# Attention stage: instruction orders of all five engines rewritten around one head pair, with two value products instead of three

## The chip, the cores and the metric

One core of a Trainium2 chip runs the whole program; the metric is the device time of one execution in microseconds. TensorE appears as PE (its weight loads as PEld), VectorE as DVE, ScalarE as ACT, GpSimd as POOL and SyncE, which only issues DMAs here, as SP. A difference counts where it is larger than 0.2%.

## The reference

The program is attention with a score threshold, a mixture of experts and a token-mixing layer, one after the other. The change is in the attention alone (4 batches x 8 heads, 576 tokens, 64 features a head):

```python
scores = scale * np.matmul(q, k.transpose(0, 1, 3, 2))
thresh = np.max(scores, axis=-1, keepdims=True) - tau
scores = np.where(scores >= thresh, scores, -1000000000.0)
scores = scores - np.max(scores, axis=-1, keepdims=True)
attn = np.exp(scores)
attn = attn / (np.sum(attn, axis=-1, keepdims=True) + 1e-09)
return np.matmul(attn, v).astype(np.float32)
```

## The kernel before

The 32 heads are worked as 16 pairs of two heads. A pair has nine tiles of 128 query rows by 576 keys: u = 0 to 7 are four full blocks of each head in turn, and u = 8 holds the last 64 rows of both heads. Each tile passes through these steps.

- **scores** (L459, PE): q and k are split into a high and a low part that are stacked along the 128 rows of the array, so that a tile is four products of 288 columns (eight in the tile of both heads). The result lies in one of three PSUM places `s_bank`. A tile may be written only when the mask of the tile three before it is done (`s_mask`).
- **row_max** (L376, DVE), **exp** (L514, ACT, into `e_ring`, two buffers), **mask** (L391, DVE, into `p_ring`, nine tiles, with the row's sum).
- **sum_eps** and **recip** (L404, L409, DVE) turn three tiles' sums into factors at once.
- **norm** (L320, POOL) multiplies a tile of `p_ring` by its factor.
- **"t"** (L472, PE) transposes the first 512 keys of a tile; **"k"** (L476, PE) transposes the last 64 keys, four tiles (or one) in a group, with 64 other keys that are thrown away; ACT copies the result (L546) into `p_t`.
- **"pv"** (L483, PE) multiplies by v: query columns 0 to 255, 256 to 511, and the last 64 in a third product. **"r"** (L488, PE) turns the result to token rows and multiplies by the gates; ACT copies it to `x_tmp`, and SP writes it out.

The groups "t", "k", "pv", "r" share two PSUM banks in turn, so each waits until the group two before it has been copied (`s_free`).

The stacked operands come by a path of their own, one pair ahead of their use. POOL scales and splits q and k of pair p+2 in five parts that stand between the norms of pair p (`split`: L292 scale, L303 and L306 high and low part of q, L311 and L314 of k). SP waits for the low parts and then copies them inside SBUF into `q_st` (`stack_q`, four copies, L193) and `k_st` (`stack_k`, four copies, L200). The first tile of scores of pair p+2 waits for all eight.

The order on each engine is fixed in the code. A step k of the loop body issues scores k+7, exp k+6, mask and row maximum near k+6, norm k+5 and the groups of tile k; the same rule serves every tile. During the last pairs POOL also splits eight pieces of the first expert's weights (`split_piece`, L53 and L55).

## Time and profile before

| | us |
|---|---|
| median of 3 runs | 906.8 (906.3 to 906.98) |
| profiled execution: time, span | 913.87, 912.1 |
| attention, from the start to the last copy of logits | 327.1 |
| PE busy in the span | 820.3 (90%) |
| 100 to 250 us: PE, DVE, ACT, POOL busy | 148.60, 117.50, 114.95, 94.67 of 150 |

The median stands 7.1 us, or 0.8%, below the profiled execution; differences are taken inside the trace and put on the median. In a timeline row the columns are the start, the time from there to the end of the last instruction merged into the row, engine and line, the operation with its operands, the count, and in brackets the idle time ahead of it and what ended it. PE matmuls overlap, so from one group's start to the next group's start is what a group costs; the row's own time is longer. In a row of stretches the columns are the stretch, its length, the busy time of PE, PEld, DVE, ACT and POOL with their counts, the granted clock, the share of the 16 DMA engines and GB/s. Names in the rows follow memory: `xs_nat` and `u` are also the places of the value result.

### The profile page before, as it was taken

The numbers are of one execution on the slowest core, as the hardware profiler recorded it, in microseconds if no ns is written. First come the engines' busy times: TensorE is split into PE (matmuls) and PEld (weight loads), VectorE is DVE, ScalarE is ACT, GpSimd is POOL, SyncE is SP. The second block draws the span as 40 slices with busy tenths as digits, with TensorE's granted clock in tenths as the row PEclk, the third lists the DMA queues.
The fourth block names the chain that finished last, engine by engine and source line by source line (L and its number), as shares of the span: only waits on it lengthen the run. The fifth ranks groups of instructions, "written<-read, shape, count | busy, mean of one in ns | idle before, by whom it ended". The sixth has DMA issues, their size and how long they took to land. (4 is left out here: it accounts for less than half of the span.)

```text
span 912.1 us, 17390 instructions
## 1 busy us (share of the span) xinstructions
PE 820.3 (90%) x5424; PEld 696.5 (76%) x5425; DVE 448.8 (49%) x1044; ACT 395.4 (43%) x669; POOL 519.8 (57%) x462
## 2 busy tenths in 40 slices
PE   1989999999999832989999999999578999999998
PEld 1778887888888621767888888888457899999998
DVE  3867877778777445112121221122156865656622
ACT  2667777778777540111222121222066634434400
POOL 3556665666588901963799779999238522503200
PEclk9899999999999975998999999999779999999999
DMA  9977567756766151675655545572121110110101
GB/s 225 327 172 176 145 157 177 177 144 167 175 151 159 56 198 56 221 226 188 230 184 173 184 138 175 181 266 73 51 89 41 36 64 19 41 53 1 37 16 52
DMA packets 81441, 123.17 MB, mean 135 GB/s; under 512 B 28352, under 2 KB 41920, under 8 KB 81408
## 3 DMA queue, kind: packets, MB, share of 16 engines
q1 hardware_dynamic: 71280, 99.34, 37.7%
q10 hardware_dynamic: 6656, 12.13, 4.2%
q0 software_dynamic: 3472, 11.28, 4.1%
q8 instruction: 19, 0.31, 0.1%
q14 instruction: 14, 0.11, 0.0%
HBM read 70.55 MB, written 23.86 MB: 103 GB/s over the span
## 5 line engine op out<-in xcount | busy, mean ns | idle before, releaser
L320 POOL TENSOR_SCALAR p_ring<-p_ring,rsum 128x576 f32<-128x576 f32 x144 | 107.1, 750 | 93.4 <-DVE rsum L409 93.2
L459 PE MATMUL psum<-k_st,q_st 128*128 128x288 f32 x640 | 125.0, 323 | 26.5 <-DMA q_st<-q_split 17.3
L376 DVE TENSOR_REDUCE negmax<-psum 128x1 f32<-128x576 f32 x144 | 108.4, 753 | 73.6 <-PE psum L459 72.4
L459 PEld LDWEIGHTS psum<-k_st,q_st 128*128 128x128 f32 x640 | 94.3, 198 | 39.3 <-issue 26.8
L997 PE MATMUL psum<-w_split,h_hi 128*128 x352 | 118.3, 408 | 4.1 <-DVE h_lo L1061 3.2
L976 PE MATMUL psum<-w_split,x_hi 128*128 x352 | 118.2, 407 | 4.1 <-issue 2.2
L391 DVE SCALAR_TENSOR_TENSOR p_ring<-psum,thresh,e_ring 128x576 f32<-128x576 f32 x144 | 116.8, 811 | 5.0 <-PE psum L476 2.3
L903 POOL TENSOR_TENSOR w_split<-w_raw,w_split 128x1024 fp32r<-128x1024 f32 x48 | 115.4, 2403 | 4.0
L514 ACT ACTIVATE e_ring<-psum,negmax 128x576 f32<-128x576 f32 x144 | 107.7, 748 | 19.3 <-DVE negmax L376 16.4
L546 ACT COPY p_t<-psum 128x512 f32<-128x512 f32 (+1 forms) x192 | 107.7, 561 | 16.1 <-PE psum L472 12.2
L472 PE MATMUL psum<-ident,p_ring 128*128 128x128 f32 x576 | 89.0, 278 | 4.5 <-POOL p_ring L320 4.0
L483 PE MATMUL psum<-p_t,v_sb 128*64 128x256 f32 (+1 forms) x960 | 89.3, 332 | 0.5 <-ACT p_t L546 0.5
L1183 POOL TENSOR_TENSOR stage<-g,xs_nat 128x512 f32<-128x512 f32 (+1 forms) x20 | 27.3, 1366 | 108.5 <-ACT xs_nat L1389 108.5
L1316 PE MATMUL psum<-tok_hi,z_hi 128*128 128x288 f32 x288 | 86.2, 299 | 1.5 <-DVE z_lo L1226 1.5
L1316 PE MATMUL psum<-tok_lo,z_hi 128*128 128x288 f32 x288 | 84.9, 295 | 0.0
L1316 PE MATMUL psum<-tok_hi,z_lo 128*128 128x288 f32 x288 | 84.8, 294 | 0.0
L1030 ACT CAST h_hi<-psum 128x1024 fp32r<-128x1024 f32 x22 | 22.4, 1017 | 142.1 <-PE psum L985 125.0
L997 PEld LDWEIGHTS psum<-w_split,h_hi 128*128 128x128 f32 x352 | 68.5, 195 | 18.9 <-issue 4.8
L976 PEld LDWEIGHTS psum<-w_split,x_hi 128*128 128x128 f32 x352 | 67.7, 193 | 18.9 <-issue 4.9
L483 PEld LDWEIGHTS psum<-p_t,v_sb 128*64 128x64 f32 x960 | 54.2, 137 | 28.0 <-ACT p_t L546 7.8
L472 PEld LDWEIGHTS psum<-ident,p_ring 128*128 128x128 f32 x576 | 67.9, 141 | 9.2 <-issue 4.8
L997 PE MATMUL psum<-w_split,h_lo 128*128 x176 | 70.8, 402 | 0.0
(182 smaller groups left out, 1563.1 us busy)
## 6 DMA issues: line engine op xcount, KB each, us to landing
w_raw<-w_dram SPq DMA_DIRECT2D x48, 512.0 KB, 3.6
k_st<-k_split SPq DMA_DIRECT2D x64, 288.0 KB, 5.0
q_st<-q_split SPq DMA_DIRECT2D x60, 144.0 KB, 2.5
xs_dram<-stage SPq DMA_DIRECT2D x23, 256.0 KB
xs_nat<-xs_dram ACTq DMA_DIRECT2D x22, 256.0 KB
ys_dram<-y_nat ACTq DMA_DIRECT2D x22, 256.0 KB, 2.1
k_nat<-k_t_dram SPq DMA_DIRECT2D x16, 288.0 KB, 4.3
q_nat<-q_t_dram SPq DMA_DIRECT2D x16, 288.0 KB, 4.6
```

Source lines behind the costliest of these rows:

```text
L320: pl.tensor_scalar(t, t, rsum[:, k % BODY:k % BODY + 1], 1.0, ALU.mult, ALU.mult).then_inc(s_norm, 1)
L376: dve.tensor_reduce(negmax[:, k % 3, 0:1], s_bank[k % 3][:, :, 0:HALF], AX.XY, ALU.max, negate=True).then_inc(s_max, 1)
L391: dve.scalar_tensor_tensor(out=p_ring[:, k % RING, :].rearrange("p (a b) -> p a b", a=2), in0=s_bank[k % 3][:, :, 0:HALF], scalar=thresh[: ...
L459: mm = pe.matmul(bank[:, x, 0:HALF], lhs, key[:, HALF * x:HALF * x + HALF], start=(j == 0), stop=(j == len(terms) - 1))
L472: mm = pe.transpose(bank[:, t * P:t * P + P], p_ring[:, k % RING, t * P:t * P + P], ident[:])
L483: mm = pe.matmul(bank[D * h:D * h + D, 0:n], v_sb[m % 2][:, h, t, :], p_t[arg % 2][:, h, t, 0:n], start=(t == 0), stop=(t == KT - 1))
L514: act.activation(e_ring[:, k % 2, :].rearrange("p (a b) -> p a b", a=2), s_bank[k % 3][:, :, 0:HALF], ACT.Exp, bias=negmax[:, k % 3, 0:1], ...
L546: act.copy(dst, src).then_inc(s_free, 1)
L903: lo = pl.tensor_tensor(w_lo[:, (m + 1) % 2, r // 4, part], raw[:, r % 4, :], w_hi[:, (m + 1) % 2, r // 4, part].bitcast(F32), ALU.subtract)
L976: mm = pe.matmul(ph[:, half, :], a[:, c, :], rhs.rearrange("p o n -> p (o n)"), start=(n == 0), stop=(n == len(terms) - 1))
L997: mm = pe.matmul(py, a[:, f, :], rhs.rearrange("p o n -> p (o n)"), start=(n == 0), stop=(n == len(terms) - 1))
L1316: mm = pe.matmul(mix_bank(b, q), a[:, k, c * P:c * P + P], w[:, k, half], start=(t == 0 and i == 0), stop=(t == ST - 1 and i == len(terms) ...
```

## The change

The order of every engine is written out for one pair (`pair(i, m)`), instead of a step that serves every tile.

- The tile of both heads' last rows is now u = 0 and comes first. Its queries join columns 0 to 255, so "pv" is one product of 320 columns and one of 256, and one copy less.
- The keys of head 0's tiles start 64 places later in memory, and tiles of both heads lie next to each other in `p_ring`. One transposition of 128 columns takes the last 64 keys of head 0 and of head 1. A pair has six "k" transpositions in two groups instead of nine in three. The last row block of v is padded with zeros for the other head.
- For this k comes with its last 64 keys repeated ahead: `k_nat`, `k_split` and `k_st` have 640 columns instead of 576. The k split on POOL, the load of k and the four stack copies grow by one ninth.
- `e_ring` has three buffers. Small tiles, `turn` and `x_t` move to memory that other stages use later.
- The weight pieces stand at other places in POOL's last four pairs.

```diff
-    e_ring = sb("e_ring", [P, 2, S], F32)
+    e_ring = sb("e_ring", [P, 3, S], F32)
-    k_st = [sb(f"k_st{m}", [P, 2, 2, S], F32R) for m in range(2)]
+    k_st = [sb(f"k_st{m}", [P, 2, 2, REM + S], F32R) for m in range(2)]
-    k_split = sb("k_split", [P, 2, S], F32R)
+    k_split = sb("k_split", [P, 2, REM + S], F32R)
+    ORDER = (("t", 0), ("pv", 1), ("t", 1), ("t", 2), ("t", 3), ("r", 1), ("k", 0), ("t", 4), ("t", 5), ("pv", 0),
+             ("k", 1), ("t", 6), ("r", 0), ("t", 7), ("t", 8))
+    BEHIND = (("pv", 1), ("r", 1))
...
+        def values(i, m, a):
+            bank = bank_of(i, m, "pv", a)
+            if a == 0:
+                pe.wait_ge(s_v[m % 2], 64 * i + 64)
+            for t in range(KT):
+                for h in range(2):
+                    moving = p_t[a][:, h, t, :] if t < FULL else p_k[a]
+                    mm = pe.matmul(bank[D * h:D * h + D, 0:COLS[a]], v_sb[m % 2][:, h, t, :], moving,
+                                   start=(t == 0), stop=(t == KT - 1))
+            mm.then_inc(s_filled, 1)
...
+            if parts:
+                split(i + 1, m, 1)
+            piece(0)
+            if here:
+                norm(i, m, 5)
+            if parts:
+                split(i + 1, m, 2)
+            if here:
+                norm(i, m, 6)
+                norm(i, m, 7)
+            if parts:
+                split(i + 1, m, 3)
+            piece(1)
+            if here:
+                norm(i, m, 8)
+            if parts:
+                split(i + 1, m, 4)
...
+            if u < 2 and not (isinstance(i, int) and 2 * i + m == 0):
+
+                dve.wait_ge(s_filled, (number(i, 0, "k", 0) if m else number(i - 1, 1, "k", 0)) + 1)
...
+        pair(ITER - 2, 0, pieces=((2, 0),))
+        pair(ITER - 2, 1, pieces=((2, 1),))
+        pair(ITER - 1, 0, pieces=((0, 2), (1, 3), (2, 4)))
+        pair(ITER - 1, 1, ahead=False, pieces=((0, 5), (1, 6), (2, 7)))
```

POOL, in the loop, from the high part of q of pair p+2 to the low part of its k; the rows on `p_ring` are norms, and the first norm after L306 is the one that needs the last factors of pair p. Before:

```order
L303 TENSOR_SCALAR q_split<-u 128x576 [waits s_qst1]
L277 REGISTER_ALU
L320 TENSOR_SCALAR p_ring<-p_ring,rsum 128x576 [waits s_rsum]
L306 TENSOR_TENSOR q_split<-u,q_split 128x576 [waits s_qhi]
L320 TENSOR_SCALAR p_ring<-p_ring,rsum 128x576 [waits s_rsum]
L311 TENSOR_SCALAR k_split<-k_nat 128x576 [waits s_kraw0,s_kst1]
L320 TENSOR_SCALAR p_ring<-p_ring,rsum 128x576 [waits s_rsum]
L314 TENSOR_TENSOR k_split<-k_nat,k_split 128x576 [waits s_khi]
```

The same place now:

```order
L307 TENSOR_SCALAR q_split<-u 128x576 [waits s_qst0]
L324 TENSOR_SCALAR p_ring<-p_ring,xs_nat 128x576 [waits s_rsum]
L310 TENSOR_TENSOR q_split<-u,q_split 128x576 [waits s_qhi]
L281 REGISTER_ALU
L324 TENSOR_SCALAR p_ring<-p_ring,xs_nat 128x576 [waits s_rsum] x2
L315 TENSOR_SCALAR k_split<-k_nat 128x640 [waits s_kraw1,s_kst0]
L324 TENSOR_SCALAR p_ring<-p_ring,xs_nat 128x576 [waits s_rsum]
L318 TENSOR_TENSOR k_split<-k_nat,k_split 128x640 [waits s_khi]
```

In the first list the norm ahead of L306 is tile 6 and waits for the pair's last factors; in the second it is tile 5, so the low part of q no longer stands behind them. Three norms and both parts of k still do.

DVE at the turn from one pair to the next, where the last three factors of a pair are made (`sums`, `rsum`, `negmax` and `thresh` are all named `xs_nat` after the change). Before, from the row maximum of the next pair's first tile:

```order
L376 TENSOR_REDUCE negmax<-psum 128x1 [waits s_scores]
L391 SCALAR_TENSOR_TENSOR p_ring,sums<-psum,thresh,e_ring 128x576 [waits s_thr,s_exp]
L381 TENSOR_REDUCE thresh<-negmax 128x1 [waits s_max]
L375 REGISTER_ALU
L376 TENSOR_REDUCE negmax<-psum 128x1 [waits s_scores]
L404 TENSOR_REDUCE rsum<-sums 128x3 [waits s_mask]
L390 REGISTER_ALU [waits s_thr,s_exp]
L391 SCALAR_TENSOR_TENSOR p_ring,sums<-psum,thresh,e_ring 128x576 [waits s_filled]
L408 REGISTER_ALU
L409 RECIPROCAL rsum<-rsum 128x3 [waits s_sum]
```

Now:

```order
L405 TENSOR_REDUCE xs_nat<-psum 128x1 [waits s_scores]
L420 SCALAR_TENSOR_TENSOR p_ring,xs_nat<-psum,xs_nat,e_ring 128x576 [waits s_thr,s_exp]
L410 TENSOR_REDUCE xs_nat<-xs_nat 128x1 [waits s_max]
L419 ISA [waits s_thr,s_exp]
L420 SCALAR_TENSOR_TENSOR p_ring,xs_nat<-psum,xs_nat,e_ring 128x576 [waits s_filled]
L430 TENSOR_REDUCE xs_nat<-xs_nat 128x3 [waits s_mask]
L404 REGISTER_ALU
L405 TENSOR_REDUCE xs_nat<-psum 128x1 [waits s_scores]
L434 REGISTER_ALU
L435 RECIPROCAL xs_nat<-xs_nat 128x3 [waits s_sum]
```

The next pair's first mask, which waits for a "k" group on PE (`s_filled`), has moved ahead of the second row maximum, and the reciprocal now stands behind both.

PE from the first tile of scores of the next pair to the "k" group for which that mask waits, as it is now:

```order
L516 MATMUL psum<-k_st,q_st 128x288 [waits s_mask,s_kst0,s_qst0]
L516 MATMUL psum<-k_st,q_st 128x288 x7
L534 MATMUL psum<-ident,p_ring 128x128 [waits s_norm,s_free]
L534 MATMUL psum<-ident,p_ring 128x128 x3
L563 MATMUL psum<-u,stage 128x137 [waits s_free]
L563 MATMUL psum<-u,stage 128x137 x2
L516 MATMUL psum<-k_st,q_st 128x288 [waits s_mask]
L516 MATMUL psum<-k_st,q_st 128x288 x3
L545 MATMUL psum<-ident,p_ring 128x128 [waits s_norm,s_free]
L545 MATMUL psum<-ident,p_ring 128x128 x3
```

The eight products of the first tile carry the waits for `k_st` and `q_st`; before the change that tile had four, and its first mask did not stand behind a "k" group that comes later than its own scores.

## Rows read from the trace of the kernel before

**Rows 1.** Busy time by stretch, the steady middle of the attention.

```profile
100.00:250.00 150.00, 148.60 (x1300) 122.87 (x1299) 117.50 (x351) 114.95 (x216) 94.67 (x124) 1.00 0.68 166
```

**Rows 2.** Timeline of PE, parts of one pair; 197.92 and 215.96 open pairs.

```profile
197.92 0.77 PE L459 MATMUL psum<-k_st,q_st 128*128 128x288 f32 x4
...
199.40 0.77 PE L459 MATMUL psum<-k_st,q_st 128*128 128x288 f32 x4
200.01 0.60 PE L472 MATMUL psum<-ident,p_ring 128*128 128x128 f32 x4
200.44 0.60 PE L476 MATMUL psum<-ident,p_ring 128*128 128x128 f32 x4
...
209.49 2.38 PE L483 MATMUL psum<-p_t,v_sb 128*64 128x256 f32 x20
...
212.62 0.80 PE L483 MATMUL psum<-p_t,v_sb 128*64 128x64 f32 x20
...
213.77 1.30 PE L459 MATMUL psum<-k_st,q_st 128*128 128x288 f32 x8
214.91 0.86 PE L488 MATMUL psum<-turn,xs_nat 128*128 x6
215.60 0.60 PE L472 MATMUL psum<-ident,p_ring 128*128 128x128 f32 x4
215.96 0.77 PE L459 MATMUL psum<-k_st,q_st 128*128 128x288 f32 x4
```

**Rows 3.** Timeline of SP: the last of four copies to k_st.

```profile
209.88 1.50 SPq L200 DMA_DIRECT2D k_st<-k_split  x1
```

**Rows 4.** Instructions on k_st, 195 to 216 us: landing of its four copies.

```profile
DMA to landing us min/median/max: 3.1/4.7/5.5
```

**Rows 5.** Timeline of POOL in the same pair.

```profile
202.23 0.75 POOL L320 TENSOR_SCALAR p_ring<-p_ring,rsum 128x576 f32<-128x576 f32 x1 [2.17 <-DVE rsum L409]
...
205.06 0.68 POOL L311 TENSOR_SCALAR k_split<-k_nat 128x576 fp32r<-128x576 f32 x1
205.71 0.75 POOL L320 TENSOR_SCALAR p_ring<-p_ring,rsum 128x576 f32<-128x576 f32 x1
206.43 1.42 POOL L314 TENSOR_TENSOR k_split<-k_nat,k_split 128x576 fp32r<-128x576 f32 x1
```

**Rows 6.** Timeline of DVE in the same pair.

```profile
201.06 0.15 DVE L404 TENSOR_REDUCE rsum<-sums 128x3 f32<-128x6 f32 x1
201.12 0.81 DVE L391 SCALAR_TENSOR_TENSOR p_ring<-psum,thresh,e_ring 128x576 f32<-128x576 f32 x1
...
201.86 0.17 DVE L409 RECIPROCAL rsum<-rsum 128x3 f32<-128x3 f32 x1
...
215.11 0.76 DVE L376 TENSOR_REDUCE negmax<-psum 128x1 f32<-128x576 f32 x1 [0.72 <-PE psum L459]
215.78 0.81 DVE L391 SCALAR_TENSOR_TENSOR p_ring<-psum,thresh,e_ring 128x576 f32<-128x576 f32 x1
```

**Rows 7.** Timeline of PE: first scores of pairs 2, 3 and 15.

```profile
52.66 0.79 PE L459 MATMUL psum<-k_st,q_st 128*128 128x288 f32 x4 [3.15 <-DMA k_st<-k_split]
...
71.64 0.80 PE L459 MATMUL psum<-k_st,q_st 128*128 128x288 f32 x4 [0.77 <-DMA k_st<-k_split]
...
288.91 0.78 PE L459 MATMUL psum<-k_st,q_st 128*128 128x288 f32 x4
```

**Rows 8.** Timeline of POOL: one weight piece, and the attention's last instruction.

```profile
300.59 1.04 POOL L53 TENSOR_SCALAR w_split<-stage 128x1024 fp32r<-128x1024 f32 x1
...
304.06 0.74 POOL L320 TENSOR_SCALAR p_ring<-p_ring,rsum 128x576 f32<-128x576 f32 x1
...
326.88 0.23 POOL L325 COPY lg<-x_tmp 128x45 f32<-128x45 f32 x1 [9.01 <-ACT x_tmp L546]
```

**Rows 9.** Timeline of PE: a long wait near the end.

```profile
300.04 0.63 PE L472 MATMUL psum<-ident,p_ring 128*128 128x128 f32 x4 [1.55 <-POOL p_ring L320]
```

**Rows 10.** Busy time by stretch, just after that wait.

```profile
300.50:304.00 3.50, 3.50 (x18) 2.95 (x18) 2.35 (x7) 2.50 (x4) 3.42 (x3) 0.51 0.02 5
```

More of the change, by code:

```diff
@@ L332, in pool @@
             split(0, 1, part)
-        for k in range(AHEAD_M):
-            norm(0, k)
-        def step(i, k, more=True, last=False, piece=None):
-            m, u = k // TILES, k % TILES
-            if u < PARTS and (m < 2 or more) and not last:
-                split(i + (m + 2) // 2, m % 2, u)
-            if piece is not None:
-                split_piece(pl, w, feed, 0, piece)
-            if not (last and k + AHEAD_M >= BODY):
-                norm(i, k + AHEAD_M)
-            for m in range(2):
-                if k == TILES * m + TILES + 4:
-                    take_logits(i, m, ALL_GROUPS - PER_ITER * i if last and m == 1 else ROWS_DONE[m])
@@ L406, in recip @@
[L406 to L422 removed]
+                out=p_tile[u].rearrange("p (a b) -> p a b", a=2), in0=s_bank[u % 3][:, :, 0:HALF],
@@ L491, in tensor, with bank_of @@
-        pe.wait_ge(s_zero, 4)
-        for k in range(AHEAD_S):
-            scores(0, k)
-        def step(i, k, groups, last=False):
-            if not (last and k + AHEAD_S >= BODY):
-                scores(i, k + AHEAD_S)
-            for n, what, arg, m in groups[k]:
-                group(i, n, what, arg, m, k)
+        def bank_of(i, m, what, arg):
+            n = number(i, m, what, arg)
+            if not (isinstance(n, int) and n < 2):
+                last = isinstance(n, int) and n >= ALL_GROUPS - len(BEHIND)
+                pe.wait_ge(s_free, n if last else n - 1)
+            return misc[number(0, 2 + m % 2, what, arg) % 2] if not isinstance(n, int) else misc[n % 2]
@@ L501, in tensor @@
+        pe.wait_ge(s_zero, 5)
+        pair(-1, 1, past=False, here=False)
         pe.wait_ge(s_ident, 16)
         pe.wait_ge(s_turn, 16)
[L503 to L546 removed]
@@ L1571 @@
     q_t = inputs["q"].transpose(0, 1, 3, 2).reshape(pairs, 2, 64, SEQ)
+    k_t = inputs["k"].transpose(0, 1, 3, 2).reshape(pairs, 2, 64, SEQ)
     gates = np.concatenate([inputs["moe_w_gate"], inputs["moe_w_local"]], axis=1).reshape(DC, P, EXPERTS + 1)
```

529 lines of the change are left out of this document (324 added, 205 removed).

## The prediction

> **What bounds the kernel now.** I read the busy times by stretch first. In the steady middle PE is busy 148.60 of 150 us, the next engine 117.50 [rows 1], so PE's order sets the pace there. The attention is over at 327.1 us (326.88 + 0.23) [rows 8]; nothing behind it is touched, so the whole effect lies ahead of that point. Busy PE rows overlap, so I then read the timeline of one pair from start to start. Pairs open at 197.92 and 215.96: a pair takes 18.04 us [rows 2].
>
> What PE needs for a pair when nothing waits follows from the steps there: a tile of scores 0.61 (199.40 to 200.01), the tile of both heads 1.14 (213.77 to 214.91), a "t" group 0.36 ahead of scores and 0.43 ahead of another group, a three-block "r" 0.69 [rows 2]. A value product of 256 columns takes 2.38 and one of 64 columns 0.80 in time busy, their steps about 0.07 less [rows 2]. Before, that is 8 x 0.61 + 1.14 + 9 x 0.38 + "k" 0.85 + "r" 1.15 + values 2 x 2.31 + 0.73 = 16.8. So 1.2 us of the 18.04 are hand-overs between engines.
>
> The second thing to see is the path on which a pair's operands come, though hardly a wait stands on it now. The low part of k is done at 207.85 (206.43 + 1.42) [rows 5]. The last of the four copies to k_st is issued at 209.88 [rows 3] and lands 5.5 us later [rows 4], at 215.38. The pair opens at 215.96. The slack is about 0.5 us in 18. From the split's end to the landing it is 7.53 us.
>
> **The change on PE.** Values become 320 and 256 columns. From 0.80 and 2.38 a column costs 0.0082 us, so 320 columns take 2.31 + 0.52 = 2.83, and the two 5.14 instead of 5.35: 0.2 saved. "k" groups have six transpositions instead of nine: 0.25 saved. PE's need falls to 16.35 us. The new order puts scores between groups wherever a bank must be copied. I walked it through with the steps above, with copies of 0.6 on ACT and 0.74 for a mask: no wait on PE over 0.3 us at any place but one. By PE alone a pair would take about 16.6 us. The third exponential buffer, the smaller key copies and one copy less on ACT, which is busy 114.95 of 150 [rows 1], are behind PE: nothing. Their cover is ACT's idle quarter; without it the copies would be on the path at 0.3 us a pair.
>
> **The place where it stays: a loop through the operands.** I count from the first tile of scores of pair p+1. All steps are in the new order, with durations of before.
> - The scores' tile of both heads now comes first. Its row maximum starts 1.34 later (213.77 to 215.11) [rows 2, 6].
> - PE goes on: "t" at 1.14, "r" of three blocks at 1.57, scores at 2.27, the four-transposition "k" group at 2.88, done 0.60 later [rows 2]. The first mask waits for this group, whose reading it would overwrite: 3.54 with the hand-over. By its own inputs it could start at 3.1.
> - Mask 0.74 (201.12 to 201.86), small sum 0.06, row maximum 0.67 (215.11 to 215.78) [rows 6]: the reciprocal that frees the last three factors of pair p starts at 5.03. POOL's norm follows 0.37 after its start (201.86 to 202.23) [rows 5, 6]: 5.40.
> - POOL now has two norms at 0.72 (205.71 to 206.43), the high part of k at 0.65, longer by a ninth, 0.73, a norm 0.72, the low part 1.42, longer by a ninth, 1.58 [rows 5]: 9.87. The waiting norms hold up the split behind them, and with it SP's copies.
> - The copies take 7.53 for 576 columns. Landings run from 3.1 after the first issue (made at 207.87, as soon as the split ends) to 215.38: 4.4 us for three copies, 1.47 each [rows 3, 4]. A ninth on four is 0.65. The q copies, which now come earlier because the low part of q stands ahead of the waiting norm, no longer share the queue in the first microsecond: back up to 0.65. I take a net +0.3: 7.8 (bounds 7.5 and 8.2).
> - With 0.1 for the last hand-over the next pair opens 17.8 us after this one (17.5 to 18.2).
>
> The same sum for before: first norm of the last three at 4.31 (197.92 to 202.23) [rows 2, 5], split done at 9.93, copies 7.53, hand-over 0.1: 17.56, just under the 18.04 that PE takes. So the change takes PE's part from 18.04 to 16.6, finds the loop at 17.8, and PE will stand about 1.2 us at each pair's first scores. Gain: 0.24 us a pair.
>
> For the longer copies the nearest page speaks for less. By the Trainium skill, DMA: Bandwidth & Descriptors, section Where 436 GB/s comes from, copies inside SBUF are bounded by a fabric of 435 GB/s; the ninth (131 KB) would then take 0.3 us rather than 0.65. Rows 4 decide, with 288 KB in 1.47 us, which is 200 GB/s counted once.
>
> **Ends.** Start: pair 2 opens at 52.66 after 3.15 us of waiting for k_st [rows 7], since everything loaded by then shares the queue. Three stacks of k longer by 0.65 and four loads of k longer by a ninth come ahead of it, 0.65 to 2.3 us. I take +1.5; nothing that PE saves in the first two pairs survives this wait. Pair 3 opens at 71.64, after another wait for k_st [rows 7]; it follows pair 2 by the same loop in both kernels, 19 us. Middle: from 71.64 to 288.91 are 12 pairs in 217.3 us [rows 7]; 12 x 17.8 = 213.6: -3.7. End: from 288.91 to 327.1 are 38.2 us. A weight piece costs POOL 3.47 (300.59 to 304.06) [rows 8]. Now from the last pair's opening PE needs 11.7 to the eighth tile's scores; POOL's piece 4 ends at 16.65, and behind it stand five norms, two more pieces and another norm until the last: 16.65 + 6 x 0.72 + 2 x 3.47 = 27.9. On that norm hang the second "k" group and four more groups (2.9, with their copies), the value product with its copy (3.0), "r" with its copy and the logits (1.7 to 2.2): 36.0, and 0.4 for a clock that may have fallen. 38.2 - 36.4 = -1.8.
>
> Sum: +1.5 - 3.7 - 1.8 = -4.0, inside the trace 912.1 to 908.1; on the median 906.8 - 4.0 = 902.8, and I say 903.
>
> **Rivals.**
> - *A, the forecast, 0.52.* Loop of 17.5 to 18.05 us; 899 to 907.
> - *B, the loop is not closed, 0.20.* If the copies land in under 7 us, or the norms come earlier than I walked, PE sets the pace. At 16.6: 12 x 1.2 = 14.4 more, 888.5. For it: the walk has steps of 0.1 to 0.4 that could shrink. Against it: every large term is a measured row. Half way (17.2) is 895.5.
> - *C, slower, 0.17.* The same loop, 18.3 us or more, where it exceeds what PE took before. It decides from 18.2: 12 x 0.5 more than A is 909. The copies at their bound of 8.2 and the mask 0.1 later suffice. For it: at pair 3 the wait came even with the shorter copies [rows 7]. Against it: the queue is free of q copies.
> - *D, the clock, 0.11.* After one wait of 1.55 us [rows 9] the granted clock stood at 0.51, the level of 1.2 GHz, for 3.5 us [rows 10]; with every group at twice its length that costs up to 1.7 us. The wait of 3.15 us at pair 2 was followed by none. If PE stands 1.2 us in each pair, the clock may fall again and again; only what exceeds PE's slack of 1.2 us a pair, and what lies in the loop's first 3.5 us, counts: about 0.9 each. From four falls it undoes the gain; in all twelve pairs it gives 903 + 11 = 914. The Trainium skill, TensorE: Matmul & The Clock Gate, section A second HAM failure mode, says that frequent short idle times between groups can make the clock swing between both levels: that speaks for D. The trace agrees in one place of three.
> - That the two value products alone bring nothing is part of A: 0.45 us less PE work a pair is invisible while the loop sets the pace.
>
> **How the numbers follow.** The likeliest is A at 903, own range 899 to 907. Faster than before by over 0.2%, which is 1.8 us and about what a measurement can tell, means under 905.0: 0.40 of A's 0.52, all of B, 0.02 of C and D: 0.62. Within 0.2%: 0.10 of A, 0.08 of C and D: 0.18. Slower: 0.20. From 889 to 910 about 0.15 is left out, half of it B at full strength, half D and the far end of C.
>
> **What the new profile would show.** Right: a pair opens every 17.8 us; ahead of its first scores PE stands about 1.2 us, put down to the DMA of k_st; the busy share of PE falls to about 92%; the value row has 320 columns at about 2.9 us. The first norm of a pair's last three starts 5.4 us after the next pair's opening, the low part of k ends at 9.9, the last copy lands at 17.7. Wrong, by B: no DMA wait there and 16.6 a pair. By C: the same wait with 18.2 or more. By D: the granted clock at 0.5 in the middle slices. What would upset the sum most is a term of the loop that I have 0.3 us wrong, since it counts 12 times.

## The result: 0.4% slower, and the profile after

Before 905.84 us (11 runs, 903.3 to 909.1), after 908.76 us (11 runs, 906.2 to 912.4); the ratio is 1.0038 [1.0021, 1.0056]. I had said 903.

Two executions of later experiments that stand far outside the others (957.6 us in experiment 2, 2523.9 us in experiment 14) are left out of every time and ratio below.

The profiled execution of the changed kernel took 909.75 us (span 907.9). It is shorter than the profiled one of before (913.87), though the medians stand the other way: behind the last copy of logits the profiled execution of before took 585.0 us and this one 577.4. Spans of single executions don't tell a difference of this size here. The stage that was changed does: its last copy of logits ends at 330.48 instead of 327.11 [rows 8], 3.4 us later, and the medians differ by 2.9. So I compare the traces up to that point.

The busy times by stretch of the changed kernel, with the columns of [rows 1]:

```profile
100.00:250.00 150.00, 142.19 (x1101) 115.60 (x1098) 117.31 (x351) 112.39 (x216) 97.76 (x127) 1.00 0.71 171
```

PE is busy 142.19 of 150 us instead of 148.60. So its busy time did shrink by 4%, and the time did not. Where it stands idle is in the list of PE's waits from 60 to 290 us (releaser; total us, times, longest):

```profile
PE psum L516 <- DMA k_st<-k_split: 10.8, 11, 1.0
PE psum L516 <- DVE p_ring L420: 1.1, 1, 1.1
```

PE waits 1.0 us once in each pair, on the stacked copy of k, ahead of the first scores. I call the start of a pair's first scores its opening. The timeline of PE over one pair and at its ends:

```profile
183.16 1.32 PE L516 MATMUL psum<-k_st,q_st 128*128 128x288 f32 x8 [1.01 <-DMA k_st<-k_split]
...
199.65 0.60 PE L534 MATMUL psum<-ident,p_ring 128*128 128x128 f32 x4
201.16 1.32 PE L516 MATMUL psum<-k_st,q_st 128*128 128x288 f32 x8 [0.92 <-DMA k_st<-k_split]
```

A pair takes 18.0 us here, and 18.06 as a mean over the nine pairs from 92.83 to 255.38: what it took before [rows 2]. PE is ready at 200.08 (199.65 and a "t" group's 0.43), 16.9 us after the opening. DVE, POOL and SP in the same pair:

```profile
184.52 0.76 DVE L405 TENSOR_REDUCE xs_nat<-psum 128x1 f32<-128x576 f32 x1 [1.21 <-PE psum L516]
...
186.62 0.82 DVE L420 SCALAR_TENSOR_TENSOR p_ring<-psum,xs_nat,e_ring 128x576 f32<-128x576 f32 x1 [0.55 <-PE psum L545]
...
187.44 0.75 DVE L405 TENSOR_REDUCE xs_nat<-psum 128x1 f32<-128x576 f32 x1
188.10 0.17 DVE L435 RECIPROCAL xs_nat<-xs_nat 128x3 f32<-128x3 f32 x1
```

```profile
188.47 1.47 POOL L324 TENSOR_SCALAR p_ring<-p_ring,xs_nat 128x576 f32<-128x576 f32 x2 [3.18 <-DVE xs_nat L435]
189.91 0.72 POOL L315 TENSOR_SCALAR k_split<-k_nat 128x640 fp32r<-128x640 f32 x1
190.61 0.74 POOL L324 TENSOR_SCALAR p_ring<-p_ring,xs_nat 128x576 f32<-128x576 f32 x1
191.32 1.55 POOL L318 TENSOR_TENSOR k_split<-k_nat,k_split 128x640 fp32r<-128x640 f32 x1
```

```profile
188.53 2.43 SPq L200 DMA_DIRECT2D q_st<-q_split  x4
192.90 3.80 SPq L207 DMA_DIRECT2D k_st<-k_split  x4
```

The four copies to k_st by themselves, the last of which is issued at 195.1 and lands 5.8 us later:

```profile
L207 SPq DMA_DIRECT2D k_st<-k_split x4: 462/803/1601, 192.9 to 195.1; - x4
DMA to landing us min/median/max: 3.3/5.0/5.8
```

Read as one chain: first scores 183.16, row maximum, first mask (0.55 late, because it waits for the "k" group L545), row maximum, reciprocal 188.10, norm 188.47 (POOL had stood 3.18 us), k's low part done 192.87, first k copy issued 192.90, last one landed 200.93, next opening 201.16. It is the loop that the prediction walked. Term by term, from the opening (the last three rows are lengths):

| | forecast | measured |
|---|---|---|
| row maximum | 1.34 | 1.36 |
| first mask | 3.54 | 3.46 |
| reciprocal | 5.03 | 4.94 |
| norm | 5.40 | 5.31 |
| low part of k done | 9.87 | 9.71 |
| copies | 7.8 | 8.06 |
| hand-over | 0.1 | 0.23 |
| pair | 17.8 | 18.0 |

The start and the end, on PE and POOL:

```profile
55.24 2.26 PE L516 MATMUL psum<-k_st,q_st 128*128 128x288 f32 x8 [3.51 <-issue]
...
74.71 1.32 PE L516 MATMUL psum<-k_st,q_st 128*128 128x288 f32 x8 [0.94 <-DMA k_st<-k_split]
...
291.91 1.30 PE L516 MATMUL psum<-k_st,q_st 128*128 128x288 f32 x8 [1.14 <-issue]
...
302.98 0.41 PE L545 MATMUL psum<-ident,p_ring 128*128 128x128 f32 x2 [1.84 <-POOL p_ring L324]
...
315.71 0.63 PE L534 MATMUL psum<-ident,p_ring 128*128 128x128 f32 x4 [1.71 <-POOL p_ring L324]
...
321.32 0.66 PE L545 MATMUL psum<-ident,p_ring 128*128 128x128 f32 x2 [2.14 <-POOL p_ring L324]
```

```profile
330.26 0.22 POOL L329 COPY lg<-x_tmp 128x45 f32<-128x45 f32 x1 [5.47 <-ACT x_tmp L668]
```

Against before (52.66, 71.64, 288.91 in [rows 7]) pair 2 opens 2.6 us later, pair 3 3.1 later, the twelve pairs to the last opening take 217.2 instead of 217.3, and from there to the end it is 38.6 instead of 38.2. That is 3.1 - 0.1 + 0.4 = 3.4 us.

### The profile page after: what moved, and what is told of

The parts are those of the page before. It is cut to its first block and busy times, and to the rows that moved or that the text cites. A ratio compares the mean times of both kernels' runs of the same rounds, so it can differ in the third digit from the quotient of the medians.

```text
span 907.9 us, 16449 instructions
## 1 busy us (share of the span) xinstructions
PE 803.6 (89%) x5056; PEld 680.7 (75%) x5057; DVE 448.8 (49%) x1044; ACT 389.0 (43%) x669; POOL 520.7 (57%) x461
## 5 line engine op out<-in xcount | busy, mean ns | idle before, releaser
L324 POOL TENSOR_SCALAR p_ring<-p_ring,xs_nat 128x576 f32<-128x576 f32 x144 | 106.0, 747 | 99.0 <-DVE xs_nat L435 99.0
L516 PE MATMUL psum<-k_st,q_st 128*128 128x288 f32 x640 | 126.3, 327 | 38.1 <-DMA q_st<-q_split 18.2
L405 DVE TENSOR_REDUCE xs_nat<-psum 128x1 f32<-128x576 f32 x144 | 105.8, 750 | 63.3 <-PE psum L516 63.2
L516 PEld LDWEIGHTS psum<-k_st,q_st 128*128 128x128 f32 x640 | 94.6, 199 | 53.2 <-issue 36.3
L420 DVE SCALAR_TENSOR_TENSOR p_ring<-psum,xs_nat,e_ring 128x576 f32<-128x576 f32 x144 | 114.6, 812 | 15.4 <-PE psum L545 8.4
L1153 PE MATMUL psum<-w_split,h_hi 128*128 x352 | 115.9, 401 | 3.2 <-DVE h_lo L1217 3.2
L628 ACT ACTIVATE e_ring<-psum,xs_nat 128x576 f32<-128x576 f32 x144 | 105.6, 750 | 20.8 <-DVE xs_nat L405 19.9
L646 ACT COPY p_t<-psum 128x512 f32<-128x512 f32 x144 | 84.5, 587 | 46.9 <-PE psum L534 44.1
L1132 PEld LDWEIGHTS psum<-w_split,x_hi 128*128 128x128 f32 x352 | 67.2, 191 | 16.6 <-issue 2.5
L534 PEld LDWEIGHTS psum<-ident,p_ring 128*128 128x128 f32 x576 | 70.7, 144 | 7.9 <-issue 5.8
L555 PE MATMUL psum<-p_t,v_sb 128*64 128x256 f32 (+1 forms) x512 | 69.1, 412 | 0.7 <-ACT p_t L646 0.7
L1132 PE MATMUL psum<-w_split,x_lo 128*128 x176 | 69.3, 394 | 0.0
```

The source lines that it names most:

```text
L324: pl.tensor_scalar(t, t, rsum[:, col:col + 1], 1.0, ALU.mult, ALU.mult).then_inc(s_norm, 1)
L405: dve.tensor_reduce(negmax[:, u % 3, 0:1], s_bank[u % 3][:, :, 0:HALF], AX.XY, ALU.max, negate=True).then_inc(s_max, 1)
L420: dve.scalar_tensor_tensor(out=p_tile[u].rearrange("p (a b) -> p a b", a=2), in0=s_bank[u % 3][:, :, 0:HALF], scalar=thresh[:, u % 3:u % 3 ...
L516: mm = pe.matmul(bank[:, x, 0:HALF], lhs, key[:, HALF * x:HALF * x + HALF], start=(j == 0), stop=(j == len(terms) - 1))
L534: mm = pe.transpose(bank[:, t * P:t * P + P], keys[:, t * P:t * P + P], ident[:])
L555: mm = pe.matmul(bank[D * h:D * h + D, 0:COLS[a]], v_sb[m % 2][:, h, t, :], moving, start=(t == 0), stop=(t == KT - 1))
```

## The experiments

Two theories were to be told apart. **L**: the operand loop sets the pace, and what PE saves turns into a wait at its end. **P**: PE and its hand-overs set 18.06, and the wait for k_st only takes the place of others. Beside them Q (the full DMA queue makes the start late) and E (norms behind weight pieces make the end late).

"Pace" is the mean distance of the pairs' openings over 8 to 11 pairs of the middle, "end" the end of the last copy of logits in the trace (before 327.1, after 330.5), the ratio is to the kernel before, run on the same chip. Before took 915.2 us in the group of the first four runs and 905.4 to 906.5 in the others, so I compare ratios, not times. Ratios of the first group must be read with care: experiments 1 and 7 end the attention at the same point, and their ratios are 0.9828 and 0.9861.

| | pace | end | us | ratio |
|---|---|---|---|---|
| before | 18.04 | 327.1 | 905.8 | 1 |
| after | 18.06 | 330.5 | 908.8 | 1.0038 [1.0021, 1.0056] |
| 1 k's split early | 16.82 | 315.8 | 900.3 | 0.9828 [0.9795, 0.9860] |
| 2 reciprocal early | 17.55 | 322.2 | 908.9 | 0.9934 [0.9909, 0.9960] |
| 3 dose, after | 19.89 | 355.2 | 943.4 | 1.0316 [1.0264, 1.0369] |
| 4 dose, before | 19.35 | 348.6 | 934.3 | 1.0204 [1.0162, 1.0246] |
| 5 zeros late | 18.05 | 327.9 | 906.5 | 1.0010 [0.9997, 1.0023] |
| 6 pieces spread | 18.06 | 338.7 | 916.8 | 1.0123 [1.0100, 1.0147] |
| 7 three edits | 16.82 | 315.8 | 893.8 | 0.9861 [0.9839, 0.9883] |
| 8 before, k early | 18.04 | 328.2 | 905.4 | 0.9997 [0.9981, 1.0012] |
| 9 pieces behind | 18.10 | 328.7 | 906.5 | 0.9998 [0.9981, 1.0014] |
| 10 k copies of 576 | 17.39 | 319.9 | 896.5 | 0.9898 [0.9871, 0.9926] |
| 11 all edits | 16.82 | 309.9 | 887.0 | 0.9780 [0.9764, 0.9797] |
| 12 before, same edits | 18.03 | 323.5 | 901.3 | 0.9945 [0.9930, 0.9959] |
| 13 logits first | 16.82 | 302.6 | 886.9 | 0.9794 [0.9769, 0.9818] |
| 14 k group first | 17.74 | 326.6 | 904.2 | 0.9976 [0.9962, 0.9991] |

### 1. k's split ahead of the waiting norms

```diff
             if parts:
                 split(i + 1, m, 2)
+                split(i + 1, m, 3)
+                split(i + 1, m, 4)
             if here:
                 norm(i, m, 6)
                 norm(i, m, 7)
-            if parts:
-                split(i + 1, m, 3)
             piece(1)
             if here:
                 norm(i, m, 8)
-            if parts:
-                split(i + 1, m, 4)
```

> The changed kernel with one edit: on POOL both parts of k's split stand ahead of the three norms that wait for the last factors, right behind the low part of q. Theory L (the operand loop sets the pace): POOL stands 3.18 us at that place, so the split fits in and ends near 4.5 us after the pair's opening instead of 9.7. SP is then bound by its own four q copies, which end at 7.8, so the first k copy goes out 1.9 us earlier and the last lands at 15.9. PE needs 16.9 for its own part, so a pair opens every 16.9 to 17.1 us, the wait ahead of its first scores is gone, and the time falls by 12 to 14 us, to about 895. Rival P (PE and its hand-overs set 18.06, the wait for k_st merely takes the place of others): other waits on PE grow by the 1.0 us, a pair stays at 18.0 to 18.1 and the time is that of the changed kernel, within 1 us. Rival C (the clock or queue contention): in between, 17.4 or more a pair, with q copies and k copies longer.

The pace falls to 16.82 us. The whole list of PE's waits from 60 to 290 us is now

```profile
PE psum L543 <- POOL p_ring L324: 1.4, 1, 1.4
PE psum L532 <- POOL p_ring L324: 0.4, 1, 0.4
```

and no wait for k_st is left. From 100 to 250 us PE is busy all the time, so 16.82 us is what PE's own order takes. POOL in one pair, which opens at 192.50:

```profile
194.46 1.43 POOL L310 TENSOR_TENSOR q_split<-u,q_split 128x576 fp32r<-128x576 f32 x1
195.87 0.72 POOL L315 TENSOR_SCALAR k_split<-k_nat 128x640 fp32r<-128x640 f32 x1
196.78 1.55 POOL L318 TENSOR_TENSOR k_split<-k_nat,k_split 128x640 fp32r<-128x640 f32 x1 [0.18 <-POOL k_split L315]
198.31 2.19 POOL L324 TENSOR_SCALAR p_ring<-p_ring,xs_nat 128x576 f32<-128x576 f32 x3
```

The split is over 5.8 us after the opening instead of 9.7 (4.5 expected), in time in which POOL stood before. Nothing was made cheaper: two instructions moved ahead of three. Rival P would have kept 18.06; it falls. Ratio 0.983 instead of 1.004 is 19 us, 5 more than expected. In the trace the end came 14.7 us earlier, close to the 12 to 14 expected. The rest was not saved behind the attention, which took 582.0 us there and 577.4 in the trace of the changed kernel. It may lie in this group's own before (915.2 us against 905.8), of which no trace was kept; in the group of experiment 7 the same end of the attention is worth 16 us.

### 2. The reciprocal ahead of the row maximum

```diff
             if past:
                 sum_eps(b_i, b_m, 2)
+                recip(b_i, b_m, 2)
             if here:
                 row_max(i, m, 1)
-            if past:
-                recip(b_i, b_m, 2)
```

> The changed kernel with one edit: on DVE the reciprocal of a pair's last three factors stands right behind their small sum, ahead of the row maximum of the next pair's second tile (0.67 us). Theory L: the norm that waits for it, and with it the split of k, its copies and the next opening come 0.55 to 0.67 us earlier: 17.4 to 17.5 us a pair, PE's wait for k_st falls from 1.0 to about 0.4, and the time falls by 7 to 9 us, to about 900. Rival P: no change of the pace, within 1 us. If the small sum's hand-over to the reciprocal is longer than I take it (0.2 us), the gain is 5 to 6.

The pair that opens at 178.78 has its reciprocal at +4.41 instead of +4.94:

```profile
183.19 0.18 DVE L435 RECIPROCAL xs_nat<-xs_nat 128x3 f32<-128x3 f32 x1
```

That is 0.53 earlier, and the pace falls by 0.51. The wait for k_st halves to 5.6 us in twelve pairs. One place exchanged on an engine that is busy 117 of 150 us moved the whole kernel by 1% (8.3 us in the trace).

### 3 and 4. The same dose on both kernels

```diff
             if part == 3:
...
                 pl.tensor_scalar(k_split[:, 0, :], k_nat[m][:], 1.0, 1.0, ALU.mult, ALU.mult).then_inc(s_khi, 1)
+                for more in (2, 1):
+                    hold(s_khi, 6 * i + 3 * m + 1 - more)
+                    pl.tensor_scalar(k_split[:, 0, :], k_nat[m][:], 1.0, 1.0, ALU.mult, ALU.mult).then_inc(s_khi, 1)
```

> The changed kernel with POOL doing the high part of k's split three times instead of once, one behind the other; nothing else. Each costs 0.73 us and a hand-over of some 0.05, so the low part ends 1.5 to 1.6 us later. Theory L: the loop passes all of it on: 19.6 us a pair, PE's wait for k_st 2.5 us, and the time grows by 14 times 1.55 = 21 to 22 us, to about 930. Rival P (POOL has a third of its time free): at most 0.6 us a pair, that is under 8 us in all.

> The kernel before with the same dose: high part of k's split three times, which adds 2 x 0.65 and two hand-overs, 1.35 to 1.4 us. By the slack of 0.5 us that I read there, the first half microsecond is free and the rest appears: 18.9 us a pair, about 0.9 more, 12 to 13 us in all, to about 919. If the path of k had far more slack than I read, there is no change; if it was already on the path, 19 us more. The difference between the two doses is what tells whether the change moved the pace from PE to this loop.

POOL's rows give the real dose. After:

```profile
204.13 0.72 POOL L315 TENSOR_SCALAR k_split<-k_nat 128x640 fp32r<-128x640 f32 x1
205.05 0.72 POOL L318 TENSOR_SCALAR k_split<-k_nat 128x640 fp32r<-128x640 f32 x1 [0.20 <-POOL k_split L315]
205.96 0.72 POOL L318 TENSOR_SCALAR k_split<-k_nat 128x640 fp32r<-128x640 f32 x1 [0.19 <-POOL k_split L318]
```

It is 1.83 us (204.13 to 205.96), the hand-over being 0.2 and not 0.05. The pace grew by 1.83: all of it. PE's wait for k_st is 1.6 us and not the 2.5 expected, because PE now also waits 1.0 us a pair for a norm that the dose delays. Before:

```profile
218.51 0.68 POOL L311 TENSOR_SCALAR k_split<-k_nat 128x576 fp32r<-128x576 f32 x1
219.39 0.67 POOL L314 TENSOR_SCALAR k_split<-k_nat 128x576 fp32r<-128x576 f32 x1 [0.20 <-POOL k_split L311]
220.25 0.68 POOL L314 TENSOR_SCALAR k_split<-k_nat 128x576 fp32r<-128x576 f32 x1 [0.19 <-POOL k_split L314]
```

Here the dose is 1.74 us and the pace grew by 1.31. The difference, 0.43, is the slack that the operand path had before, if what exceeds it passes on in full, as it did after; the prediction had read 0.5 from the landing and the next opening. The change used it up. Both expectations were low mainly because the dose was larger than I took it.

### 5. The zeros out of the start

```diff
-        extra(sp)
...
         pair(BATCH - 1, 1)
+        extra(sp)
```

> The changed kernel with one edit: ten copies that fill parts of two DRAM tables with zeros (256 KB each), which SP issues at 32.5 to 38.4 us, go out after the last stack copies instead (during the fourteenth pair), and the constants of the routing with them. Theory Q (what the start loses is the full DMA queue): from the first k copy for pair 2 to its last landing it is 10.7 us, in the steady middle 8.1; without the 2.6 MB pair 2 opens 2.5 to 3 us earlier, the granted clock does not fall there (it stood at 0.51 from 55 to 58 us, behind a wait of 3.5 us), and pair 3 follows after 18.1 us instead of 19.5. Together 3.5 to 4.5 us less, about 905 against 908.8; the middle stays at 18.06 a pair. Rival: the queue is full of loads of q, k, v and weights anyway, and only 0 to 1 us comes back. What the zeros cost near the end, where the queue is a quarter busy, I take as nothing.

Pair 2 opens at 52.69 (2.6 earlier) with 1.2 us of waiting instead of 3.5, pair 3 at 70.57 (4.1 earlier); the granted clock from 51 to 58 us is 1.00. In the changed kernel it was 0.51 just behind the long wait, and the eight products of 55.24 took 2.26 us instead of 1.32:

```profile
55.00:58.00 3.00, 2.76 (x12) 2.78 (x13) 0.47 (x1) 0.00 (x0) 0.00 (x0) 0.51 0.46 97
```

Theory Q holds at the start. At the end part of it is lost: the last pair opens 19.0 us after the one before (1.8 of it a wait), and from there to the end it is 39.8 instead of 38.6. That the zeros in their new place cost this is not shown. In experiment 9, where they stand in the old place, the last pair also opens 18.9 us after the one before; and in this execution the granted clock fell near the end, where it was 0.97 over the corresponding 10 us of the changed kernel:

```profile
308.00:318.00 10.00, 7.11 (x36) 4.84 (x38) 1.57 (x7) 3.56 (x8) 9.83 (x10) 0.66 0.12 35
```

Net 2.6 us in the trace and 0.28% in the ratios, where 3.5 to 4.5 us were expected.

### 6 and 7. Weight pieces in earlier pairs

```diff
-        pair(ITER - 2, 0, pieces=((2, 0),))
-        pair(ITER - 2, 1, pieces=((2, 1),))
-        pair(ITER - 1, 0, pieces=((0, 2), (1, 3), (2, 4)))
-        pair(ITER - 1, 1, ahead=False, pieces=((0, 5), (1, 6), (2, 7)))
+        pair(ITER - 2, 0, pieces=((0, 0), (2, 1)))
+        pair(ITER - 2, 1, pieces=((0, 2), (2, 3)))
+        pair(ITER - 1, 0, pieces=((0, 4), (2, 5)))
+        pair(ITER - 1, 1, ahead=False, pieces=((0, 6), (2, 7)))
```

> The changed kernel with one edit: POOL's eight weight pieces stand two in each of the last four pairs (ahead of the norm that waits for the last factors, and behind the first norms of the next pair) instead of 1, 1, 3 and 3. Theory E (the end is lost on norms behind pieces): PE waited 1.8, 1.7 and 2.1 us for norms after 302 us; with one piece less ahead of them in the last pair, two of the three waits shrink, 3.5 us less in the end. Against it the pieces ahead of the waiting norm fill POOL's idle 3.18 us and exceed it by 0.3, and the loop is longer by 0.3 to 1.0 us in three pairs: 1 to 2 us more. Net 1.5 to 2.5 us less. Rival: the pieces in earlier pairs cost the loop as much as they free at the end, no change.

A miss: 8.2 us later at the end, where 1.5 to 2.5 us less were expected. I had looked at POOL's time and not at its data. The fifth piece is loaded into a place that the first must have freed, and SP issues that load only after the fourteenth pair. POOL stood in the sixth experiment

```profile
POOL w_split L53 <- DMA stage<-w_dram: 9.7, 1, 9.7
```

and behind it the norms for which PE then waited 7.8 us. The seventh run (edits 1 and 5, with one piece in each of the last eight pairs, and their loads moved ahead by pairs) fell into the same hole:

> The changed kernel with three edits: k's split ahead of the waiting norms (as in the first experiment), the zeros late, and one weight piece in each of the last eight pairs, behind the last norms of the pair and ahead of the first of the next, where POOL now stands 2.9 us. If the parts add up: 15 less from the start of the trace's before (the first experiment alone against before), 3 to 4 more from the start (pair 2's wait and the clock behind it), 3 to 5 more from the end (waits of 1.4, 1.7 and 2.1 us for norms behind pieces): ratio to before about 0.975, that is 22 us less than before. Rival: the pieces (3.5 us in a gap of 2.9) delay the first norms by 0.6 us and PE's first groups on them, so that 0.5 us a pair over eight pairs eats the gain of the end: 18 less than before.

Its pace is 16.82, pair 2 opens at 51.31 without a wait, but one piece waited 8.9 us for its weights, and PE 8.0 for a norm behind it. So its end is that of the first experiment, and its ratio of 0.986 misses the 0.975 expected.

### 8. Control: the same early split without the change

```diff
-            if u < PARTS and (m < 2 or more) and not last:
-                split(i + (m + 2) // 2, m % 2, u)
+            if u < 2 and (m < 2 or more) and not last:
+                for part in ((0,), (1, 2, 3, 4))[u]:
+                    split(i + (m + 2) // 2, m % 2, part)
```

> Control: the kernel before with k's split moved in the same way, ahead of the norm that waits for the last factors. Theory L: before, the pace is PE's own (18.04 us with its hand-overs), the operand path had 0.4 us of slack, so the middle stays at 18.0 to 18.05 a pair; only pair 2's and pair 3's openings can come earlier, by 0 to 2 us. Ratio 0.998 to 1.0. If instead the early split is a gain in itself, whatever PE's order, it shows here as well: 16.9 a pair, 13 us less.

No change, 18.04 a pair and a ratio of 0.9997. Pairs 2 and 3 don't open earlier either. The kernel before was set by PE's order with its hand-overs, the kernel after is set by the operand loop. That both take 18.05 us is a coincidence. The cleanest price of the early split is the pair of experiments 1 and 8, which move the same two parts: 16.82 against 18.04 a pair, and an end of 315.8 against 328.2.

### 9. The last pieces behind the norms

```diff
-        pair(ITER - 1, 1, ahead=False, pieces=((0, 5), (1, 6), (2, 7)))
+        pair(ITER - 1, 1, ahead=False, pieces=((2, 5), (2, 6), (2, 7)))
```

> The changed kernel with one edit: the last pair's three weight pieces stand behind its last norm on POOL, not ahead of and between them. Theory E (the end is lost on norms that stand behind pieces): PE waits there 1.8, 1.7 and 2.1 us; without these the last norms end 10 us sooner and the attention ends 4.5 to 5.5 us sooner, measured from the last pair's opening (38.6 now). The pieces end at about 25 us after that opening instead of 29, so nothing behind them is later. The time falls by 4 to 5.5 us, to 904 against 908.8. Rival: the waits move to the copies of ACT and to the granted clock (which falls near there anyway), and only 1 to 2 us come back.

The two waits of the last pair (1.7 and 2.1) are gone, and from its opening to the end it is 36.3 us instead of 38.6; the opening itself came 0.5 later. The time went down by 0.40%, 3.6 us, a little less than the 4 to 5.5 expected. Of the 3.9 us of waits 2.3 came back: hand-overs from ACT of 0.5, 0.2 and 0.2 us, which those waits had covered, are now seen, and in this execution the granted clock was 0.83 from 300 to 310 us.

### 10. What the ninth of the bytes costs

```diff
-                    sp.dma_start(k_st[m][half * D:half * D + D, h, :, :].bitcast(F32),
-                                 k_split[h * D:h * D + D, :, :].bitcast(F32)).then_inc(s_kst[m], 16)
+                    sp.dma_start(k_st[m][half * D:half * D + D, h, :, :].rearrange("p a s -> p (a s)")[:, 0:2 * S].bitcast(F32),
+                                 k_split[h * D:h * D + D, :, :].rearrange("p a s -> p (a s)")[:, 0:2 * S].bitcast(F32)).then_inc(s_kst[m], 16)
```

> The changed kernel with one edit: each copy to k_st moves 1152 of the 1280 elements of a row, so that the four have the size of before; the rest of k_st stays zero (the last 128 places of the low part of k are left out of the scores). The split and the loads stay as long as they are. From the end of the split to the last landing it is 8.06 us now and was 7.53 before. By the price that I took for a ninth of the bytes, 0.65 us, the pace falls to 17.4 and the time by 8 to 9 us. By the 435 GB/s that the Trainium skill gives for copies inside SBUF it is 0.3 us, a pace of 17.75 and 4 us. If the copies are bound by their issue on SP or by their landing delay, the bytes cost nothing and the pace stays at 18.06. I expect 0.3 to 0.65.

(The cut leaves out that the unwritten places of k_st are set to zero at the start. This kernel leaves the last 128 columns of k's low part out of the scores, so its output differs from the reference; it serves only for the time.)

The low part of k is done at 184.13 and the last copy lands at 191.57:

```profile
182.56 1.57 POOL L320 TENSOR_TENSOR k_split<-k_nat,k_split 128x640 fp32r<-128x640 f32 x1
```

That is 7.44 us instead of 8.06, and the pace is 17.39 instead of 18.06. The ninth costs 0.62 us in these two pairs (0.68 as a mean over all pairs of the middle), close to the 0.65 that [rows 4] gave. The estimate of 0.3 us that follows from the 435 GB/s of the Trainium skill (DMA: Bandwidth & Descriptors, Where 436 GB/s comes from) doesn't hold for these copies; the added bytes went at half of that. It also tests the other half of my term: with the same bytes as before the copies take 7.44 instead of 7.53 us, so the q copies, which are issued earlier now, give back 0.1 at most and not up to 0.65. The time fell by 12.7 us, more than the 8 to 9 expected. The trace shows 10.6 of them: 7.5 in the twelve pairs and 4.6 up to pair 3, where the queue is full, less 1.6 at the end. Pair 2 opens at 52.85, 2.4 us earlier than in the changed kernel and 0.2 later than before. So the added bytes of the stack copies account for nearly all of what the start lost.

### 11. All edits

```diff
-        pair(ITER - 2, 0, pieces=((2, 0),))
-        pair(ITER - 2, 1, pieces=((2, 1),))
-        pair(ITER - 1, 0, pieces=((0, 2), (1, 3), (2, 4)))
-        pair(ITER - 1, 1, ahead=False, pieces=((0, 5), (1, 6), (2, 7)))
+        pair(ITER - 2, 0, pieces=((3, 0),))
+        pair(ITER - 2, 1, pieces=((3, 1),))
+        pair(ITER - 1, 0, pieces=((3, 2),))
+        pair(ITER - 1, 1, ahead=False, pieces=((3, 3), (3, 4), (3, 5), (3, 6), (3, 7)))
```

(Place 3 is behind a pair's last norm. Beside it stand edit 1, and `extra(sp)` ahead of SP's last pair.)

> The changed kernel with three edits: k's split ahead of the waiting norms; the zeros sent in the last pair; the weight pieces behind the norms of the last four pairs (1, 1, 1, 5). If the theories L, Q and E hold and add up: the middle at 16.82 us a pair (12 x 1.24 = 14.9), the start 4 us better (pair 2 without its wait), the end 5 us better: attention ends at about 306 us in its trace, 24 us before that of the changed kernel; against before about 21 us less, ratio 0.977. Rival: what is gained at the start is lost at the end to zeros and to the clock, and 15 to 17 us remain.

887.0 us, 0.978 of before: with that of experiment 13, which differs from it by 0.1 us, the fastest kernel here. From 100 to 250 us:

```profile
100.00:250.00 150.00, 150.00 (x1178) 123.58 (x1176) 125.32 (x377) 120.65 (x232) 107.71 (x136) 1.00 0.75 185
```

PE is busy all the time. The attention ended at 309.9 and not at 306: its last copy of logits stood behind the five pieces on POOL.

### 12. Before with the same freedom

The edit of experiment 8, and `extra(sp)` ahead of SP's last pair.

> The kernel before with the same freedom: k's split ahead of the waiting norm and the zeros sent in the last pair. It keeps its three value products, its own orders of PE, DVE and ACT, and its own places of the pieces. Theory L: its middle stays at 18.04 a pair, since PE with its hand-overs sets it; only the start gains, 2 to 4 us, ratio 0.996 to 0.998. The distance to the kernel with all edits, 17 to 19 us, is then what the change is worth once the operand loop is out of its way. If the pace falls below 17.9 here, the orders of the change aren't what brings the 16.8.

The pace stays at 18.03. The gain of 0.55% is all in the start (pair 2's last tile of scores begins at 64.73 instead of 68.43). The distance to experiment 11, 0.9945 against 0.9780, is 15 us, less than the 17 to 19 expected. It is the worth of the change once the loop is opened, together with the third edit of experiment 11: this kernel keeps its weight pieces in their old places, and their move alone was worth 3.6 us in experiment 9.

### 13. Logits ahead of the last pieces

```diff
-        pair(ITER - 1, 1, ahead=False, pieces=((3, 3), (3, 4), (3, 5), (3, 6), (3, 7)))
-        pair(ITER, 0, here=False, ahead=False)
+        pair(ITER - 1, 1, ahead=False, pieces=((3, 3), (3, 4), (3, 5)))
+        pair(ITER, 0, here=False, ahead=False, pieces=((3, 6), (3, 7)))
```

> The kernel with all edits, and the last two weight pieces behind the last copy of logits on POOL, not ahead of it. With all edits that copy (0.22 us) went out at 309.7, behind five pieces in a row, though its input was there near 302.6; so 7 us of the attention's end were POOL's. Now three pieces stand ahead of it (10.4 us, over near 302.9) and two behind. If the routing behind the attention waits for the logits, the copy goes out near 303 and the time falls by 4 to 7 us, to 880 to 883. Rival: what follows waits for the split weights and for the zeros (the DMA was full until 310), so that it only begins later and 0 to 2 us come back.

The rival is right that nothing comes back: the copy of logits went out at 302.39, 7.3 us earlier, and the time is the same. The first instruction of the routing on DVE, in the kernel with all edits and in this one:

```profile
310.56 0.07 DVE L827 MEMSET etok<- 128x20 f32 x1 [20.45 <-PEq L1628]
```

```profile
310.04 0.07 DVE L827 MEMSET etok<- 128x20 f32 x1 [20.39 <-PEq L1628]
```

Each begins 0.6 us behind POOL's last instruction, which ends at 309.94 (the copy of logits) and at 309.47 (the last piece). In the code the attention is a block of its own, which every engine leaves before the routing begins; the logits are only one of the things that it waits for. "The end" here is POOL's last instruction, in either order.

### 14. The "k" group ahead of the second tile's scores

```diff
+            if here:
+                last_keys(i, m, 0)
             if ahead:
                 scores(n_i, n_m, 1)
-            if here:
-                last_keys(i, m, 0)
-            if ahead:
                 scores(n_i, n_m, 2)
```

> The changed kernel with one edit: PE issues the first k group of a pair ahead of the scores of the next pair's second tile, not behind them. Nothing is added or taken away. Theory L with the first mask as a link: that mask starts 3.46 us after the opening, 0.55 after DVE was free, because it waits for this group; by its exponential it could start at 3.05. The group now starts when its bank has been copied, at 2.45, and ends near 3.05. So the mask, the reciprocal behind it, the norms, k's split and the copies come 0.35 to 0.4 us earlier: 17.7 us a pair, 5 us less in all, 904. Rival: the mask is not a link, since the second row maximum ahead of the reciprocal now waits for its scores (0.6 later on PE), and the pace stays at 18.06.

In the pair that opens at 181.92 the first mask starts at +3.16 instead of +3.46 and the norm at +5.01 instead of +5.31:

```profile
185.08 0.82 DVE L420 SCALAR_TENSOR_TENSOR p_ring<-psum,xs_nat,e_ring 128x576 f32<-128x576 f32 x1 [0.24 <-PE psum L545]
...
186.93 1.47 POOL L324 TENSOR_SCALAR p_ring<-p_ring,xs_nat 128x576 f32<-128x576 f32 x2 [2.56 <-DVE xs_nat L435]
```

Both are 0.30 earlier, and the pace falls by 0.32. The wait of the mask is a link of the loop. Three links, on DVE, SP's copies and PE (2, 10, 14), and a dose on POOL (3) thus each passed to the pace in full; that is what a closed loop looks like.

## Why the prediction was wrong

The mechanism of "The place where it stays" was right: PE's need fell, the loop through the operands took over, the wait stands where it was said, and the busy share fell (to 95%, not 92%). PE's own order takes 16.82 us a pair (experiments 1 and 11), not 16.6, so the wait is 1.0 us and not 1.2. What failed are sizes of the sum. The sum was -4.0 us and came out at +3.4 in the trace. The 7.4 us between them are three terms.

- **Middle, 3.6 us: "I take a net +0.3" for the copies.** From the split's end to the last landing it is 8.06 us in the pair shown (8.13 as a mean over the middle), not 7.8. The ninth was priced right at 0.65 (0.62 measured). The give-back by q copies that "no longer share the queue" was my guess, and it is 0.1 at most. With the landing's hand-over, 0.23 instead of 0.1, and 0.16 less up to the split's end, the pair shown takes 18.0 instead of 17.8; the twelve take 18.1 each. The prediction named this: a term 0.3 off counts twelve times. My bounds of 17.5 to 18.2 held the value; but they held a loop as long as before too, and I gave "faster" 0.40 of A's 0.52 all the same. Measured, the loop was 17.61 before (18.04 less the slack of 0.43) and is 18.06 now: the change lengthened it by 0.45, where I had 0.24 (17.56 to 17.8), and so ate the whole slack. The terms agree: 0.22 less up to the split's end (9.93 to 9.71), 0.53 more for the copies, 0.13 more for the hand-over than the 0.1 taken for before.
- **Start, 1.6 us: "I take +1.5" for pair 2.** It is 2.6, 0.3 beyond my upper bound of 2.3, and 0.5 more were lost up to pair 3. Experiments 5 and 10 show the cause, the added bytes in a full queue: without the zeros, or without the ninth, pair 2 opens as early as before (at 52.69 and 52.85, and at 52.66). The granted clock then fell behind the 3.5 us wait. In the profiled execution of before it did not, behind 3.15 us; in experiment 8, before with nothing but the early split, it did, behind 3.0 us. So up to 1 us of this term is a matter of which executions were profiled. Rival D had this risk in the middle, where it did not come, and not here.
- **End, 2.2 us: "36.0, and 0.4 for a clock that may have fallen".** The last norm ended 29.3 us after the last opening, not 27.9, because POOL stood 1.28 us for the last factors ahead of those norms, which the walk had left out. From there it is 9.3 us instead of 8.5, while the granted clock was 0.66 from 322 to 326 us. No run separates these two parts. Experiment 9 takes the norms out from behind the pieces and gets 2.3 us.

Rival B (PE paces) was the case that would have paid most, and one exchange on POOL makes it true, at 16.8 us a pair. Rival C (slower) put the loop at 18.3; the loop stayed at the old pace, and the loss came from the start and a little from the end. Rival D did not come in the middle: with 1.0 us of standing in every pair the granted clock from 100 to 250 us is 1.00. By the Trainium skill (TensorE: Matmul & The Clock Gate, A second HAM failure mode) frequent short idle times between groups may make the clock swing; this trace doesn't show it in the middle.

## What to carry to other kernels

When a change shortens the work of the engine that sets the pace, walk the next-longest loop through all engines and queues, and write down its slack beside the gain: here 0.43 us stood against a planned 1.4, and the change lengthened that loop too. In such a loop ask which instruction stands behind a wait that it doesn't need: k's split needed nothing of the norms ahead of it, and moving it was worth 14.7 us in the trace, where the change by itself had lost 3. Before moving work that consumes loaded data, follow the load and what frees its place, too.

## What was unexpected of the hardware

- Two instructions in a row on POOL, the second of which waits for the first one's semaphore, have 0.2 us between them (rows of experiments 1, 3 and 4).
- The length of one wait of PE does not by itself say what the clock does behind it. Of the twelve kernels in which PE waited at pair 2, ten waited 3.0 to 4.9 us. Behind nine of these waits the granted clock of the next 3 us was between 0.50 (the level of 1.2 GHz) and 0.66; behind the tenth, 3.15 us in the kernel before [rows 7], it was 1.00. Behind 2.15 us (experiment 10) and 1.17 us (experiment 5) it was 1.00 too, but one wait of 1.55 us near the end of before was followed by 0.51 [rows 9, 10]. And 1.0 us every 18 us never lowered it. Here is the same stretch in before, and in before with the early split (experiment 8), where pair 2 had waited 3.15 and 3.02 us:

```profile
53.00:56.00 3.00, 3.00 (x28) 3.00 (x26) 2.49 (x7) 1.99 (x4) 0.00 (x0) 1.00 0.40 92
```

```profile
53.00:56.00 3.00, 3.00 (x14) 3.00 (x15) 1.56 (x4) 0.48 (x2) 2.27 (x3) 0.52 0.41 80
```

- Where it fell, in the changed kernel, it made the loss of the start larger by about 1 us (eight products in 2.26 instead of 1.32).
- Four copies of 288 and 320 KB differ by 0.62 us in their last landing (0.68 as a mean over the middle): 131 KB more at 190 to 210 GB/s.
